# Two of three token blocks in table order, the third stored directly; loads issued behind the last expert's store; a longer skipped path on TensorE

## The reference

```python
def _moe_ref(x, w_gate, w1, w2, capacity) -> np.ndarray:
    ...
    h = np.maximum(np.einsum('ecd,edf->ecf', disp, w1), 0.0)
    y = np.einsum('ecf,efd->ecd', h, w2)
    ...
        if keep[i]:
            out[i] = gate_w[i] * y[expert_idx[i], pos[i]]
...
def _moe2_ref(x, w_in, w_out, a, b) -> np.ndarray:
    h = x @ w_in
    h2 = h * h
    h3 = h2 * h
    P = a[0] + a[1] * h + a[2] * h2 + a[3] * h3
    Q = 1.0 + np.abs(b[0]) * np.abs(h) + np.abs(b[1]) * h2
    g = P / (Q + 1e-06)
    return (g @ w_out).astype(np.float32)
```

## Time and profile before

| what | us |
|---|---|
| median of three runs | 565.6 |
| lowest, highest | 565.35, 566.5 |
| the profiled execution | 563.1 |
| its span, first to last instruction | 561.3 |

### The profile page before, as it was taken

How to read it: one execution, slowest core, us unless ns; L and a number is a source line. 1 busy time by engine, 2 the same in 40 slices (tenths; PEclk the granted TensorE clock), 3 DMA queues, 4 the chain that set the end, 5 groups by cost and what they waited for, 6 DMA issues and landing times.

```text
span 561.3 us, 8994 instructions
## 1 busy us (share of the span) xinstructions
PE 538.6 (96%) x3405; PEld 462.8 (82%) x3405; DVE 406.6 (72%) x742; ACT 320.7 (57%) x484; POOL 82.6 (15%) x79
## 2 busy tenths in 40 slices
PE   7999999999999999999869999999999999999983
PEld 6888889898998999989658888888888888888862
DVE  4578876564745647457559999998888888888880
ACT  3555625464644646447577776757575758565540
POOL 3433215710101101004010011004000002000002
PEclk9999999999999999999998999999999999999998
DMA  9999839869968384903330000003000001000001
GB/s 194 243 265 246 227 116 388 257 241 367 373 268 293 132 322 158 367 19 95 104 125 2 0 19 20 2 1 106 8 20 19 2 0 41 35 1 0 1 1 75
DMA packets 65424, 72.30 MB, mean 129 GB/s; under 512 B 41826, under 2 KB 42338, under 8 KB 65380
## 3 DMA queue, kind: packets, MB, share of 16 engines
q1 hardware_dynamic: 59060, 56.78, 32.6%
q0 software_dynamic: 3584, 10.51, 5.9%
q10 hardware_dynamic: 2736, 4.42, 2.1%
HBM read 59.10 MB, written 12.61 MB: 128 GB/s over the span
## 4 chain that ended last, share of the span: by engine, by line
PE 82%; DVE 6%; ACT 3%; issue 2%; DMA 2%; SPq 1%; another core or an unknown queue 1%; POOL 0%; ACTq 0%; DVEq 0%
PE bank L844 22%; PE bank L846 22%; PE bank L845 22%; PE bank L305 2%; PE bank L271 2%; PE bank L294 2%; DMA ybuf<-ysb 1%; SPq L1507 1%; PE bank L339 1%; PE bank L253 1%; PE bank L285 1%; PE bank L808 1%; DVE wa L1348 1%; DMA kin<-in_k_dram 1%
## 5 line engine op out<-in xcount | busy, mean ns | idle before, releaser
L778 DVE TENSOR_TENSOR T<-raw,T 128x1024 fp32r<-128x1024 f32 x60 | 71.6, 1223 | 50.3 <-ACT T L772 49.8
L844 PE MATMUL bank<-T,gL 128*128 128x512 f32 x192 | 75.8, 395 | 6.8 <-DVE gL L1389 6.8
L845 PE MATMUL bank<-x2L,T 128*128 128x512 f32 x192 | 74.8, 390 | 2.7 <-issue 2.7
L844 PE MATMUL bank<-x2H,T 128*128 128x512 f32 x192 | 75.5, 393 | 0.0
L845 PE MATMUL bank<-T,gH 128*128 128x512 f32 x192 | 75.4, 393 | 0.0
L846 PE MATMUL bank<-T,gH 128*128 128x512 f32 x192 | 75.3, 392 | 0.0
L846 PE MATMUL bank<-x2H,T 128*128 128x512 f32 x192 | 74.8, 390 | 0.0
L844 PE MATMUL bank<-xH,T 128*128 128x256 f32 x256 | 72.6, 284 | 0.3 <-DVE T L778 0.3
L846 PE MATMUL bank<-xH,T 128*128 128x256 f32 x256 | 72.4, 283 | 0.0
L845 PE MATMUL bank<-xL,T 128*128 128x256 f32 x256 | 72.4, 283 | 0.0
L1329 ACT ACTIVATE sq<-bank 128x512 f32<-128x512 f32 x48 | 28.5, 594 | 68.0 <-PE bank L846 60.5
(11 more groups left out here) (156 smaller groups left out, 1054.0 us busy)
## 6 DMA issues: line engine op xcount, KB each, us to landing
raw<-in_moe_w_dram SPq DMA_DIRECT2D x14, 2048.0 KB
raw<-in_moe_w_dram SPq DMA_DIRECT2D x8, 512.0 KB, 4.8
ybuf<-ysb ACTq DMA_DIRECT2D x16, 256.0 KB, 6.0
w_out_raw<-in_moe_w_out_dram SPq DMA_DIRECT2D x4, 1024.0 KB, 16.5
qin<-in_q_dram SPq DMA_DIRECT2D x12, 256.0 KB, 5.5
kin<-in_k_dram SPq DMA_DIRECT2D x12, 256.0 KB, 5.9
vin<-in_v_dram SPq DMA_DIRECT2D x12, 256.0 KB, 5.9
xbuf<-xt SPq DMA_DIRECT2D x12, 256.0 KB, 3.7
```

Source lines behind the costliest of these rows:

```text
L778: e.tensor_tensor(W[w][:, 1, cols], raws[par][:, w, cols], W[w][:, 0, cols].bitcast(F32), ALU.subtract).then_inc(r.wL[w], 1)
L844: nc.tensor.matmul(out_, aL, bH, start=start, stop=False)
L845: nc.tensor.matmul(out_, aH, bL, start=False, stop=False)
```

## The change

The table of records covers eight tiles (NMOVE = NT - TB) instead of twelve, so only the tokens of the first two blocks change places. The third block's tokens keep their order; their records are read straight from `rec`, and SP stores their tiles with plain DMAs (`sp_o`) in place of POOL's indirect ones. `seven_all` is copied for eight tiles; two operations of `dve_tables` go to `dve_order`, behind the choice of the experts. `pe_last_outs` is gone: the last three steps are done as all others. SP's loads of the later half of w_in wait for the last expert's stores instead of its matmuls. ScalarE's linear term counts on `s_w` instead of a semaphore of its own. TensorE's `redo`, in the skipped path, gets 16 small matmuls more.

```diff
+    NMOVE = NT - TB
+    table = nc.dram_tensor("table", (NMOVE * P, 4), U32, kind="Internal").ap()
...
-            e.tensor_scalar(rest_all[:, :], cc("token"), -1.0, float(NTOK - 1), ALU.mult, ALU.add).then_inc(s_const, 1)
-            e.tensor_copy(rec[:, :, 2:4], cc("token")[:, :, None].to_broadcast([P, NT, 2])).then_inc(s_const, 1)
...
-            e.tensor_copy(seven_all[:, t:t + 1], bank[7][:, 2 * E - 1:2 * E])
+            if t < NMOVE:
+                e.tensor_copy(seven_all[:, t:t + 1], bank[7][:, 2 * E - 1:2 * E])
...
+            e.wait_ge(s_pc, NMOVE)
+            e.wait_ge(s_const, 6)
+            token = cc("token")[:, 0:NMOVE]
+            e.tensor_copy(rec[:, :, 2:4], cc("token")[:, :, None].to_broadcast([P, NT, 2])).then_inc(s_gate, 1)
+            e.tensor_scalar(rest_all[:, :], token, -1.0, float(NMOVE * P - 1), ALU.mult, ALU.add).then_inc(s_gate, 1)
+            e.tensor_tensor(seven_all[:, :], token, seven_all[:, :], ALU.subtract).then_inc(s_gate, 1)
...
-            for t in range(NT):
+            for t in range(NMOVE):
                 e.indirect_dma_start(table[:, :], bass.IndirectOffsetOnAxis(ap=place_all[:, t:t + 1], axis=0),
...
+        def record(n, a):
+
+            return rec2[:, n, a:a + 1] if n < NMOVE else rec[:, n, a:a + 1]
...
-        def pe_last_outs():
-
-            e = nc.tensor
-            n = NB * FT - 1
-            e.wait_ge(s_g, n)
-            for s in range(2):
-                for m in (n - 2, n - 1):
-                    out_product(m, s)
-            e.wait_ge(s_g, n + 1)
-            for s in range(2):
-                out_product(n, s).then_inc(s_m2, 1)
-            for s in range(2, TB):
-                for m in (n - 2, n - 1):
-                    out_product(m, s)
-                out_product(n, s).then_inc(s_m2, 1)
...
         def o_ready(e, bk, s):
-            e.wait_ge(s_m2, bk * (FT - 1 + TB) + (FT if bk < NB - 1 else FT - GB + 1) + s)
+            e.wait_ge(s_m2, bk * (FT - 1 + TB) + FT + s)
...
+        def sp_o(bk):
+            e = nc.sync
+            for s in range(TB):
+                e.wait_ge(s_o[s], bk + 1)
+                dst = out.rearrange("(b t p) n -> p b t n", p=P, t=TB)[:, bk, s, :]
+                e.dma_start(dst, osb[:, s, :]).then_inc(s_end, 16)
...
-            e.wait_ge(main.mm2, NMAIN * E)
+            e.wait_ge(main.yst, 16 * NMAIN * E)
             for c in range(2, 4):
                 load_win_late(c)
+            sp_o(NB - 1)
+            for s in range(TB):
+                e.wait_ge(s_out[s], 16 * (NB - 1))
+            e.wait_ge(s_end, 16 * TB)
...
-            for s in range(TB):
-                pool_o(NB - 1, s)
-            for s in range(TB):
-                e.wait_ge(s_out[s], 16 * NB)
...
             def redo():
                 pe_x2_ready(again)
+                pe_hold(16)
                 again.finish(e)
             spilled(e, flag[0], lambda: pe_experts(spill), redo)
             blocks(pe_block)
-            pe_last_outs()
+            for n in range(NB * FT - GB, NB * FT):
+                pe_out(n)
```

More of the change, by code:

```diff
@@ L61, in build_program @@
     ybuf = nc.dram_tensor("ybuf", (YROWS, DM), F32, kind="Internal").ap()
-    table = nc.dram_tensor("table", (NTOK, 4), U32, kind="Internal").ap()
+    NMOVE = NT - TB
+    table = nc.dram_tensor("table", (NMOVE * P, 4), U32, kind="Internal").ap()
     with ExitStack() as ctx:
@@ L79, in build_program @@
         rec = sb(ctx, "rec", [P, NT, 4], U32)
-        rec2 = sb(ctx, "rec2", [P, NT, 4], U32)
-        seven_all = sb(ctx, "seven_all", [P, NT])
-        rest_all = sb(ctx, "rest_all", [P, NT])
-        place_all = sb(ctx, "place_all", [P, NT], U32)
+        rec2 = sb(ctx, "rec2", [P, NMOVE, 4], U32)
+        seven_all = sb(ctx, "seven_all", [P, NMOVE])
+        rest_all = sb(ctx, "rest_all", [P, NMOVE])
+        place_all = sb(ctx, "place_all", [P, NMOVE], U32)
         index = sb(ctx, "index", [P, E * ST], U32)
@@ L1028, in build_program @@
         s_gx, s_t2, s_x2H, s_x2L = sem("s_gx"), sem("s_t2"), sem("s_x2H"), sem("s_x2L")
-        s_m1, s_w, s_a, s_m, s_rc = (sem(n) for n in ("s_m1", "s_w", "s_a", "s_m", "s_rc"))
+        s_m1, s_w, s_m, s_rc = (sem(n) for n in ("s_m1", "s_w", "s_m", "s_rc"))
         s_p, s_hf, s_gh, s_vq, s_d, s_g, s_m2 = (sem(n) for n in ("s_p", "s_hf", "s_gh", "s_vq", "s_d", "s_g", "s_m2"))
@@ L1112, in load_wout @@
                               w_out.rearrange("(t p) n -> p t n", p=P)[:, c * n:(c + 1) * n, :]).then_inc(s, 16)
+        def record(n, a):
+            return rec2[:, n, a:a + 1] if n < NMOVE else rec[:, n, a:a + 1]
         def gather(e, buf, rows, n):
             return e.indirect_dma_start(buf[:, :], None, ybuf[0:rows, :],
-                                        bass.IndirectOffsetOnAxis(ap=rec2[:, n, 0:1], axis=0))
+                                        bass.IndirectOffsetOnAxis(ap=record(n, 0), axis=0))
         def scaled(e, buf, n):
-            return e.activation(buf[:, :], buf[:, :], ACT.Copy, scale=rec2[:, n, 1:2].bitcast(F32))
+            return e.activation(buf[:, :], buf[:, :], ACT.Copy, scale=record(n, 1).bitcast(F32))
         def turned(e, bk, buf):
@@ L1294, in pe_out @@
                     wait(e, s_o[s], bk)
-                last = out_product(n, s)
+                toks, cols = slice(s * P, (s + 1) * P), slice(f * DM, (f + 1) * DM)
+                last = three(bank[4 + s][:, :], gH[n % GB][:, toks], gL[n % GB][:, toks], T23[:, 0, cols], T23[:, 1, cols],
+                             f == 0, f == FT - 1)
                 if f == FT - 1 or s == TB - 1:
                     last.then_inc(s_m2, 1)
-        def out_product(n, s):
-            f = n % FT
-            toks, cols = slice(s * P, (s + 1) * P), slice(f * DM, (f + 1) * DM)
-            return three(bank[4 + s][:, :], gH[n % GB][:, toks], gL[n % GB][:, toks], T23[:, 0, cols], T23[:, 1, cols],
-                         f == 0, f == FT - 1)
-        def pe_last_outs():
-            e = nc.tensor
-            n = NB * FT - 1
-            e.wait_ge(s_g, n)
-            for s in range(2):
-                for m in (n - 2, n - 1):
-                    out_product(m, s)
-            e.wait_ge(s_g, n + 1)
-            for s in range(2):
-                out_product(n, s).then_inc(s_m2, 1)
-            for s in range(2, TB):
-                for m in (n - 2, n - 1):
-                    out_product(m, s)
-                out_product(n, s).then_inc(s_m2, 1)
         def act_terms(n):
@@ L1332, in act_terms @@
             wait(e, s_d, n - 1)
-            e.activation(pa[o][:, :], h[:, :], ACT.Identity, scale=ab[:, 3:4], bias=ab[:, 2:3]).then_inc(s_a, 1)
+            e.activation(pa[o][:, :], h[:, :], ACT.Identity, scale=ab[:, 3:4], bias=ab[:, 2:3]).then_inc(s_w, 1)
         def act_reciprocal(n):
@@ L1408, in pool_o @@
             e.wait_ge(s_o[s], bk + 1)
-            e.indirect_dma_start(out[:, :], bass.IndirectOffsetOnAxis(ap=rec2[:, bk * TB + s, 2:3], axis=0), osb[:, s, :],
+            e.indirect_dma_start(out[:, :], bass.IndirectOffsetOnAxis(ap=record(bk * TB + s, 2), axis=0), osb[:, s, :],
                                  None).then_inc(s_out[s], 16)
+        def sp_o(bk):
[4 more added lines that the diff above has]
+                e.dma_start(dst, osb[:, s, :]).then_inc(s_end, 16)
         AHEAD = 8
```

15 lines of the change are left out of this document (7 added, 8 removed).

## The result

The changed kernel takes 552.4 us (median of 4 runs, 551.9 to 552.8), the kernel before 565.7 beside it (565.35 to 566.5). The ratio is 0.976, 95% interval 0.975 to 0.978: 2.4% faster, 13.2 us. The forecast was 553.6 us, from 551.0 to 557.0.

What follows compares the result with a forecast made beforehand. TensorE has matmuls in 96% of the span, so only its waits and what precedes its first or follows its last matmul give time. 4.2 + 2.7 + 0.9 + 4.2 = 12.0 us off 563.1, plus 2.5: 553.6 us, range 551.0 to 557.0.

Steps and rivals of the forecast that it cites:

- Term 1: Start of last stage: with loads behind the store, ScalarE's first square comes at 279.1 instead of 283.27, 4.2 us earlier.
- the second rival: TensorE's code gap stays: square only 2.5 us earlier, clock holds, 11.7 us gained, 553.9 us; chance 0.09.
- all three conditions: Needed for the first square: the store landed (278.0 to 279.3), h(0) complete (278.0 without gap), ScalarE past its jump (276.4 to 279.8).
- The branch target: TensorE's skipped path, 16 matmuls longer, loses the 2.66 us code gap behind the jump; nothing by itself, lets h(0) meet the store.
- The clock: TensorE's clock falls again behind a 3.2 us wait for the first gL and costs the same 1.7 us: term 0.
- the first rival: The clock does not fall at the shorter wait for the first gL: 1.4 us more gained, 552.2 us; chance 0.30.
- Term 2: Last output products in plain order: last copy starts at 550.1 instead of 552.81, 2.7 us earlier.
- Terms 3 and 4: End: SP's plain last stores instead of POOL's indirect ones, 0.9 us; POOL's drain no longer at the end, 4.2 us.
- the fourth rival: The 4.8 us tail is there whoever ends last: only 7.8 us gained, 557.8 us; chance 0.07.
- The small parts: Fewer scatters and copies, smaller table, two moved VectorE operations, merged semaphore: from -0.3 to +0.1 us, taken as 0.
- The last step: The 2.5 us between the profiled 563.1 us and the median 565.6 us, carried over from 551.1 to 553.6 us.

Runs made afterwards that it cites:

- run 1: The changed kernel without the 16 extra matmuls in TensorE's skipped path: 555.0 us, ratio 0.980 to the kernel before.
- run 8: The changed kernel without the path for experts with more than 256 tokens and without its branches, on every engine: 550.8 us, ratio 0.973.
- run 5: The changed kernel with the last block's four stores by GpSimd again (indirect) and GpSimd ending last: 559.1 us, ratio 0.986.
- run 3: The changed kernel with the old order of the last three steps' output products (`pe_last_outs` called again): 556.0 us, ratio 0.980.
- run 9: The changed kernel with twelve scatters on GpSimd again, four of them to a table nobody reads: 552.6 us, ratio 0.980.
- run 10: The changed kernel with VectorE's part of the records as before (two early operations, twelve copies, wait for twelve tiles), scatters still eight: 551.5 us, ratio 0.978.
- run 6: The changed kernel itself, unaltered, measured and profiled again: 552.1 us, ratio 0.974.
- run 2: The changed kernel with SP's two w_in loads issued behind the last expert's matmuls again, not behind its stores: 555.9 us, ratio 0.980.
- run 4: The changed kernel with GpSimd waiting for the last copy before it ends, issuing no further DMA: 554.2 us, ratio 0.977.

## Why the prediction was right, and where it wasn't

**Term 1 (4.2 us): right in kind, 0.3 us too large.** Loads behind the store and the removed gap bring the square 3.9 us forward, of which the loads alone are 2.3 (8.17 to 5.83 in run 1; the second rival had 2.5 for this case). The upper part of the interval was the right choice, since all three conditions had to be met, and the one met last was ScalarE's jump: 277.9 plus 2.9 us, where the forecast had 276.4 plus at most 3.4. It read the 50 ns row rightly as not the jump's price. The remaining 0.9 us (run 8) is the price of that jump behind a store that landed after 2.4 us. Against the second and third profile of before (square 7.6 and 7.3 us behind the start) the gain is 3.4 and 3.1 us: how late the store lands behind the loads varies, 7.2, 6.7 and 6.4 us.

**The branch target: right.** The gap is gone in the changed kernel, and run 1 brings it back with 1.6 us at the end.

**The clock: the event right, the price wrong.** PE waits 3.4 us for gL (forecast 3.2) and the clock falls as before. In the experiments waits of 2.1 and 2.2 us at this place kept it at full, those of 3.0 us (run 5) and more did not; of four waits of 2.46 us at the end one was followed by a fall. But one step failed, that without the fall VectorE would be the limit for two products only, which leaves 1.4 of the 1.7 us as a gain. VectorE and not TensorE sets the pace through the first fifteen steps, and what a full clock gives TensorE it waits for VectorE at 321 us. The fall is worth 0 (0.2 to 0.9 where it lasts 6.8 us), so the first rival (552.2 us, chance 0.30) had no gain to give. That the time came out beside its figure is chance.

**Term 2 (2.7 us): right.** 2.7 in the table and 2.7 in run 3.

**Terms 3 and 4 (0.9 + 4.2 = 5.1 us): right for the sum, incomplete as reasons.** From the start of the last copy to the end it is 3.2 us instead of 8.5, 5.3 less. The store by SP was issued 0.03 us behind its copy (the forecast had 0.1, from no row) and landed in 2.0 us as taken, and GpSimd's drain begins 80 us ahead of the end. But the terms were costed one by one on the old spacing of the copies. Undone in the changed kernel they give back 6.6 us in the trace and 6.3 us in the time (ratios 0.9856 and 0.9744 of 566.6 us), since GpSimd's issue of a store each 1.27 us becomes the limit. That its drain stays whoever ends last (the fourth rival) falls: SP's is 7 ns.

**The small parts: right.** Runs 9 and 10 differ from the changed kernel by no more than it does from itself.

**The last step, the 2.5 us carried over from the median: wrong in its reason, and too large.** The forecast added the distance between the first profile of before and its median to the changed kernel's time, as if it were common to both. The changed kernel's median lies 0.3 us below its own profile (1.0 below in run 6). In the distance of before were 1.3 us or so of favourable attention, which is common to both. Beside it stand the late hH (at most 1.5 and 0.5 us more of it in the second and third profile than in the first) and in some runs the fall of the clock at the end, which the changed kernel doesn't have. So the sum from the profile, 551.1 us, needed 1.5 us because the last stage begins that much later (1.9 of attention, less 0.4 from there to the last stage), 0.1 for the terms, and -0.3 from profile to median: 552.4 us. The forecast's 553.6 is 1.2 us above, all of it from this step; and the median gained 13.2 us where the steps gave 11.9.

**What stays open** is the cause of the late hH. It isn't the scatters (run 9), VectorE's part (run 10), the placeholders (run 1), the place of the loads (run 2), the tail (run 3) or who stores last (run 5), since hH is on time in all of these. ScalarE has the same operations in the same order up to there in both kernels. What is left are, among others, the sizes of the record tables and with them the addresses behind them, the merged semaphore, or two of the parts only together. None of these was run. That it makes up most of what the median gained beyond the 11.9 us is an argument from three traces, in which it cost at most 0.3, 1.8 and 0.8 us; it isn't shown.

## What to carry to other kernels

Where an operand must make a round trip through DRAM on the critical path, hold the big loads of the same moment behind the landing of the small store, and see that neither a jump nor a gap in the code holds the engines on both sides of it. Three things had to be on time here: the loads alone gained 2.3 us, removing the gap alone gained nothing that could be told, and with both the jump was left, at 0.9 us. Ask also which engine sets the pace behind a wait before a price is put on TensorE's clock. Let the engine whose end of program is expensive end early, and cost edits of a tail together, since an issue rate that widely spaced copies had hidden becomes the bound once they come closer together. And take a second profile of the kernel before a difference between profile and median is carried into a forecast.

## What the runs showed of the hardware

- **GpSimd's drain at the end of a program** took 4.3 us behind its last stores, 4.0 us in run 5, 3.7 us with nothing in flight (run 4), and 7.8 us where it ended at 471 us with the other engines at work (10.1 us in run 8). SP's took 7 to 127 ns.
- **A taken branch** took 3.3 to 4.3 us of TensorE's queue (thirteen profiles) and 2.9 to 3.2 us of ScalarE; on ScalarE the row of the branch shows 50 ns of it, and without the branches the square came 0.85 us sooner behind the landing.
- **The branch and a store beside it**: the first of the last expert's two stores was on its way while TensorE was at its branch. It landed after 3.3 to 4.3 us, and in each of the thirteen profiles within about 0.1 us of the duration of that branch; in run 8, without branches, it took 2.0 us. What ties the two together isn't shown.
- **A 256 KB store** landed after 2.0 to 3.0 us with no load ahead of it (the last expert's second store, ten profiles), and after 5.9 to 7.2 us with 2 MB issued 0.7 us before it.
- **VectorE beside GpSimd**: one lane_hot of 0.28 us took 1.07 us when it was issued 0.07 us behind a tensor operation of GpSimd of 1.06 us (changed kernel, 49.4 us; one occurrence). At the same place in the first two profiles of before, where VectorE came first or GpSimd was done, it took 0.28 and 0.27.

```profile
49.37 1.06 POOL L576 TENSOR_TENSOR vs<-vin,cst 128x512 f32<-128x512 f32 x1 [1.93 <-PE bank L304]
49.44 1.07 DVE L483 TENSOR_SCALAR lane_hot<-cst,lane_of 128x128 f16<-128x128 f32 x1
```
